# Softmax of a tiled attention: exponentials on ScalarE from PSUM by row groups, with the maximum as bias and the sums accumulated

## The reference

```python
# q, k, v: (8, 8, 576, 64), q and k times 8
k_p = k.reshape(B, H, 72, 8, D).mean(axis=3)
v_p = v.reshape(B, H, 72, 8, D).mean(axis=3)
scores = scale * np.matmul(q, k_p.transpose(0, 1, 3, 2))      # 576 x 72 a head
scores = scores - np.max(scores, axis=-1, keepdims=True)
attn = np.exp(scores)
attn = attn / (np.sum(attn, axis=-1, keepdims=True) + 1e-09)
x = np.matmul(attn, v_p)         # -> (4608, 512), heads side by side
h = x @ w_in;   x = np.maximum(0.01 * h, h) @ w_out           # 512 -> 2048 -> 512
h = x @ w2_in;  out = (h * np.clip(h + 3, 0, 6) / 6) @ w2_out
```

## Time and profile before

| | us |
|---|---|
| median of 3 runs (1792.47 to 1794.03) | 1793.36 |
| the profiled execution, its own time | 1795.66 |
| its span, first to last instruction | 1793.9 |
| TensorE busy | 1713.4 (96%) |
| DVE busy | 1032.4 (58%) |
| ACT busy | 623.1 (35%) |
| GpSimd busy | 696.9 (39%) |

### The profile page before, as it was taken

One profiled execution on the slowest core, in us unless ns is written; L12 is line 12 of the kernel. 1 busy time (PEld: TensorE's weight loads), 2 busy tenths in 40 slices (PEclk: granted clock), 3 DMA queues, 4 the chain that ended last, 5 costly groups with the idle time before them and its releaser, 6 DMA issues. The chain is left out here.

```text
span 1793.9 us, 34434 instructions
## 1 busy us (share of the span) xinstructions
PE 1713.4 (96%) x10794; PEld 1513.2 (84%) x10794; DVE 1032.4 (58%) x1786; ACT 623.1 (35%) x1249; POOL 696.9 (39%) x773
## 2 busy tenths in 40 slices
PE   7888889999999999999999999999999999999999
PEld 7676778888888888888889888988898989888898
DVE  8664755767767677675544555444444444444444
ACT  4443333323333233333222334333433343333333
POOL 5667867666855667522220424120303030312200
PEclk8898999999999999999999999999999999999999
DMA  5744567776867768665757775766666676757562
GB/s 142 236 128 148 186 224 241 249 247 208 272 208 253 231 213 261 214 220 172 223 177 245 213 233 175 214 198 201 202 191 219 176 216 179 219 177 215 176 200 80
DMA packets 218111, 366.81 MB, mean 204 GB/s; under 512 B 22464, under 2 KB 47040, under 8 KB 218048
## 3 DMA queue, kind: packets, MB, share of 16 engines
q1 hardware_dynamic: 218048, 366.04, 65.9%
HBM read 308.28 MB, written 57.67 MB: 204 GB/s over the span
## 5 line engine op out<-in xcount | busy, mean ns | idle before, releaser
L1341 PE MATMUL ps_h<-xs_hi,ring 128*128 128x256 f32 x3808 | 819.3, 283 | 22.6 <-issue 8.5
L1341 PEld LDWEIGHTS ps_h<-xs_hi,ring 128*128 128x128 f32 x3808 | 642.2, 189 | 72.8 <-issue 37.6
L1341 PE MATMUL ps_h<-xs_lo,ring 128*128 128x256 f32 x1904 | 533.7, 280 | 0.0
L1341 PEld LDWEIGHTS ps_h<-xs_lo,ring 128*128 128x128 f32 x1904 | 359.7, 189 | 27.8
L921 ACT ACTIVATE g_hi<-gate 128x512 fp32r<-128x512 f32 x288 | 182.0, 632 | 452.9 <-DVE gate L1101 260.8
L718 POOL TENSOR_TENSOR xs_lo<-x_stage,xs_hi 128x512 fp32r<-128x512 f32 x51 | 74.8, 1466 | 464.3 <-ACT xs_hi L893 464.3
L1134 DVE TENSOR_TENSOR u<-ps_h,p 128x256 f32<-128x256 f32 x272 | 114.5, 421 | 208.4 <-PE ps_h L1341 186.9
L1293 PE MATMUL ps_y<-g_hi,wout_hi 128*128 128x512 f32 x576 | 229.3, 398 | 0.2
L1295 PE MATMUL ps_y<-g_hi,wout_lo 128*128 128x512 f32 x576 | 228.5, 397 | 0.0
L1293 PE MATMUL ps_y<-wout_hi,g_hi 128*128 128x512 f32 x576 | 226.2, 393 | 1.4 <-DVE y_stage L1130 1.4
L1295 PE MATMUL ps_y<-wout_hi,g_lo 128*128 128x512 f32 x576 | 227.0, 394 | 0.0
(11 more groups left out here) (127 smaller groups left out, 2417.9 us busy)
## 6 DMA issues: line engine op xcount, KB each, us to landing
ring<-w_in_split SPq DMA_DIRECT2D x920, 256.0 KB, 2.8
w_in_split<-ring SPq DMA_DIRECT2D x56, 256.0 KB, 4.0
w_in_split<-stage SPq DMA_DIRECT2D x56, 256.0 KB, 3.4
k_raw<-in_kT SPq DMA_DIRECT2D x32, 288.0 KB, 3.7
q_raw<-in_qT SPq DMA_DIRECT2D x32, 288.0 KB, 4.4
v_raw<-in_v SPq DMA_DIRECT2D x32, 288.0 KB
x0T<-x_stage SPq DMA_DIRECT2D x32, 288.0 KB, 4.1
x1T<-y_stage SPq DMA_DIRECT2D x36, 256.0 KB, 3.6
```

Source lines behind the costliest of these rows:

```text
L1341: mm = pe.matmul(banks[BANK_OF[r]], a, b[:, r, c, :], start=r in OPENS and c == 0 and n == 0, stop=c == 1 and n == 2, skip_group_check=True)
```

## The change

Four things. The stage exp is split in two, exp0 and exp1, one for each half, with places of their own. In them ACT reads the scores from PSUM by the six groups of 72 columns, one instruction each, with the negated and scaled maximum as bias (a pointer to one value per row), writes the exponentials to `prob`, and accumulates their sum into `row_sum`. DVE makes the bias (a small multiplication a half) in place of the subtraction, and the two row sums go. And normalize waits for both halves at once; the places of normalize, divide and turn_p0 are moved as the list says, and the wait for the earlier transposes goes from DVE to ACT.

```diff
-STAGES = ("split_qk", "scores", "exp", "normalize", "divide", "turn_p0", "pv0", "turn_p1", "pv1")
-UNIT_PLACES = [(0, 3, 4, 5, 6, 9, 11, 12, 14),
-               (11, 15, 16, 17, 18, 20, 23, 24, 26),
-               (23, 27, 28, 29, 30, 33, 35, 36, 38),
-               (35, 39, 40, 41, 42, 44, 47, 48, 50)]
+STAGES = ("split_qk", "scores", "exp0", "exp1", "normalize", "divide", "turn_p0", "pv0", "turn_p1", "pv1")
+UNIT_PLACES = [(0, 3, 4, 5, 6, 7, 9, 11, 12, 14),
+               (11, 15, 16, 17, 19, 19, 21, 23, 24, 26),
+               (23, 27, 28, 29, 30, 31, 33, 35, 36, 38),
+               (35, 39, 40, 41, 43, 43, 45, 47, 48, 50)]
...
 # FIRST_STAGES: ("exp", c) becomes ("exp0", c), ("exp1", c) in the same place of the list
...
+            u.row_bias = buf("row_bias", [ROWS, 2, HALF_SUB * 2])
...
-                if name == "exp":
-                    for half in range(2):
-                        act.wait_ge(shifted, 2 * n + half + 1)
-                        nc.scalar.activation(u.prob[:, half], u.prob[:, half], ACT.Exp,
-                                             scale=SCORE_SCALE).then_inc(exp_ready, 1)
+                if name in ("exp0", "exp1"):
+                    half = int(name[-1])
+                    act.wait_ge(bias_ready, 2 * n + half + 1)
+                    above_zero(act, p_turned, 2 * freed(b, c))
+                    for r in range(HALF_SUB * 2):
+                        rows_exp = nc.scalar.activation(
+                            u.prob[:, half, r], u.ps[0:ROWS, half, r * KEYS:(r + 1) * KEYS],
+                            ACT.Exp, bias=u.row_bias[:, half, r:r + 1], scale=SCORE_SCALE,
+                            accum_out=u.row_sum[:, half, r:r + 1])
+                    rows_exp.then_inc(exp_ready, 1)
...
-                    above_zero(dve, p_turned, 2 * freed(b, c))
                     for half in range(2):
                         dve.wait_ge(max_ready, 2 * n + half + 1)
-                        nc.vector.tensor_tensor(u.prob[:, half], scores(u, half),
-                                                spread(u.row_max[:, half]), ALU.subtract
-                                                ).then_inc(shifted, 1)
+                        nc.vector.tensor_scalar(u.row_bias[:, half], u.row_max[:, half],
+                                                -SCORE_SCALE, None, ALU.mult
+                                                ).then_inc(bias_ready, 1)
                 if name == "normalize":
-                    for half in range(2):
-                        dve.wait_ge(exp_ready, 2 * n + half + 1)
-                        nc.vector.tensor_reduce(u.row_sum[:, half], u.prob[:, half], AXIS_X,
-                                                ALU.add).then_inc(sum_ready, 1)
-                    dve.wait_ge(sum_ready, 2 * n + 2)
+                    dve.wait_ge(exp_ready, 2 * n + 2)
```

More of the change, by code:

```diff
@@ L80 @@
 STORE2_PLACES = (19, 31)
[L82 to L91, removed]
+FIRST_STAGES = [("sum_k", 0), ("sum_k", 1), ("split_qk", 0), ("split_qk", 1),
+                ("scores", 0), ("exp0", 0), ("exp1", 0), ("scores", 1), ("exp0", 1),
+                ("exp1", 1), ("normalize", 0), ("divide", 0), ("split_qk", 2),
+                ("turn_p0", 0), ("pv0", 0), ("normalize", 1), ("divide", 1), ("round", 0),
[4 rows of a table added]
+                ("normalize", 3), ("divide", 3), ("pv0", 2), ("round", 4), ("round", 5),
+                ("turn_p1", 2), ("turn_p0", 3), ("split_x", 0), ("split_x", 1), ("pv1", 2),
+                ("pv0", 3), ("round", 6), ("round", 7), ("turn_p1", 3), ("split_x", 2),
+                ("pv1", 3), ("split_x", 3)]
 WARM_UP = 8
@@ L231, in ffn_attention_kernel @@
         max_ready = sem("max_ready")
-        shifted = sem("shifted")
+        bias_ready = sem("bias_ready")
         exp_ready = sem("exp_ready")
-        sum_ready = sem("sum_ready")
         den_ready = sem("den_ready")
```

## The result

The changed kernel takes 1822.65 us (median of 3 runs, 1822.01 to 1825.31) against 1793.36 (1792.47 to 1794.03). The ratio is 1.0173, with a 95% interval of 1.0149 to 1.0197: 29.3 us slower, where 53 were forecast. The profiled execution of after took 1822.0 us, that of before 1795.7.

The account below looks back on a forecast made before the run. TensorE, busy 96% of the span, was taken to bound the kernel. Tiles 1 to 6 add 42 us, tile 0 4, before tile 0 7: 53 us on 1795.7, less 2.3, gives 1846 us; range 1789 to 1886.

Parts of the forecast that it names:

- units 1 and 3: Steps 2 and 5 of attention tiles: TensorE delayed 2.4 us each, two per tile, in tiles 1 to 6.
- h late at part 4: Steps 2 and 5: ACT's copy h stands behind exp0, so TensorE's part 4 starts 1.6 us late.
- pv0 behind the upper g_hi: Steps 2 and 5: pT_hi follows g_hi on ACT, so TensorE goes on at pv0 at 678.55 instead of 677.5.
- X: Time from one 96x72 exponential to the next on ACT: 0.44 us taken, bounds 0.24 and 0.54.
- rival A: DVE's relief decides: row sums free on ACT, X 0.24, about 8 us faster, 1785 us; chance 0.13.
- units 0 and 2: Attention tiles 1 to 6: the exponentials make copy p and TensorE's part 2 late, 1.1 us each.
- DVE's relief: Subtractions and row sums go, small multiplications come: DVE gets back 2.0 us per unit, 64 us in all.
- before tile 0: One chain of DVE, ACT and TensorE sets the pace there; ACT's longer exponentials add 7 us.
- tile 0: Delay from turn_p0 to pv0 of units 1 and 3 and later weight splitting: 4 us, between 0 and 10.
- nothing differs: Sign: from tile 7 on, the changed kernel runs as before.
- B: The second instruction, reading the sum, does not overlap: X 0.54 or a little over, 1884 us; chance 0.21.
- C: No change: X near 0.25, GpSimd's stretching merely falls on other instructions, 1793 us; chance 0.08.

Follow-up runs that it names:

- e5: The changed kernel with turn_p0 of units 1 and 3 back at its old place, one position earlier: 1809.47 us, ratio 1.0095.
- e9: The changed kernel with ACT's upper g_hi of steps 2 and 5 put behind pT_hi, as it stood before: 1812.34 us, ratio 1.0133.
- e3: The kernel before, with its own arithmetic, but normalize, divide and turn_p0 at the changed kernel's places: 1821.99 us, ratio 1.0152.
- e4: The changed kernel with exp0 of units 1 and 3 one place later, behind ACT's copy h: 1829.72 us, ratio 1.019.
- e7: The change in units 0 and 2 alone; units 1 and 3 as in the kernel before, arithmetic and places: 1797.07 us, ratio 1.003.
- e1: The kernel before with only the new buffer row_bias added, unused, shifting later allocations by 48 bytes a partition: 1794.64 us, ratio 1.0012.
- e12: The changed kernel itself, run again beside e11 for comparison: 1822.56 us, ratio 1.0184.
- e8: The kernel before without maximum and subtraction, one exponential of 96x432 a half straight from PSUM, sums on DVE: 1774.13 us, ratio 0.991.
- e10: The kernel before with one maximum for all six groups of a half as bias of one exponential from PSUM: 1780.37 us, ratio 0.9945.
- e11: The changed kernel with the first unit's row_bias at the end of the allocation, so other tensors lie as before: 1820.98 us, ratio 1.0174.
- e6: The changed kernel without the accumulator output, row_sum set once to a constant: 1806.07 us, ratio 1.0097.

## Why the prediction was right in kind and nearly twice too large

**Right in place, and in size partly by luck: units 1 and 3.** I put 2.4 us each, from h late at part 4 and pv0 behind the upper g_hi. Measured: steps 2 and 5 longer by 2.11 and 1.77 us in the mean. Both waits are there under the names foretold, h 4.6 to 13.1 us (I said over 20) and pT_lo 24.5 to 36.6 (over 35). e5 and e9 take away one link each of the second (turn_p0's place, g_hi ahead of pT_hi), and pv0's wait goes or shrinks by two thirds. e3 shows that the places make this wait without the new arithmetic, e4 that the two waits belong to one chain: remove the first, and the second takes its length.

The size came out of two errors that offset each other. With X at the measured 0.295, my own working gives part 4 at 670.4, the last exponential at 672.1, pT_lo at 676.8 and about 0.65 us a unit, not 2.4, or some 8 us in tiles 1 to 6. The term that was too small is DVE's: 0.4 us for the two small operations and 1.2 for the division. In after, of the ten places at which these precede pv0 (steps 2 and 5 of tiles 2 to 6), three have no GpSimd instruction beside them; there they take 1.6 us in all, as I put it, and pv0 waits 0.4. At the other seven they take 2.3 to 3.2 us, and pv0 waits 1.1 to 2.1. Before, they were stretched in the same way, but the chain had room, and pv0 waited at none of the ten. I used GpSimd's stretching only for rival A, and not in this chain.

**Wrong: X, and with it units 0 and 2.** The failing term is X, 0.44 foretold, 0.295 measured. I had the right instruction (a second one, of 209 ns; the nearest row had 203), but took it to stand in line with its exponential but for one neighbour's overlap. It overlaps at both ends, and adds only 0.09 us. By my own working, twelve pieces then take 3.5 us instead of 5.3, and p comes before TensorE's part 2 has use for it: units 0 and 2 cost nothing instead of 1.1 each. The wait for p stayed at 2.7 us (I said over 10), steps 1 and 4 did not grow, and e7 has these two units alone at 0.3% with the layout in it. DVE's relief was 52 us in all against my 64, since the 96x6 multiplications took 0.35 us each in the mean and not 0.2. That takes 2.2 x 6 = 13 us off the 53.

**Wrong: before tile 0 and tile 0.** 7 and 4 us foretold, 0.4 measured for both. TensorE's first matmul of tile 0 came 2.2 us late (54.3 against 52.0), and tile 0 gave back 1.8 of it; both are near the scatter (50.6 in e1, 52.1 in e12). The 7 follow X: with 0.295 my working gives about 1 (0.5 each for units 2 and 3). In tile 0 one gain repeats: the longest wait for the divided probabilities is 5.6 us in before, e1 and e3, where row_den took 2.33 to 2.35 us, and 2.8 us in after and e12, where it took 0.17. That is the wait that rival A named. e8 and e10 point the same way: in this stretch less DVE work pays. That this gain nearly cancels ACT's growth is argued; no run divides tile 0 itself.

**Not foreseen: the layout**, about 2 us from tile 7 on. I wrote "nothing differs" there. e1 and e11 show it in the matmuls' rows.

**The sum** by measured terms: 0.4 + 1.6 + 22.1 + 2.2 = 26.3 us in the profiled executions (29.3 in the medians). That the forecast came within a factor of two thus rests on an X that was too large and a DVE chain that was too short. Of the 22.1, (2.11 + 1.77) x 5 = 19.4 are of steps 2 and 5, and the rest falls on the other six. Of that rest step 3 has most (+1.00 in the mean), but in two of its five tiles it is 1.5 us and more over the others, as single steps in before are too, so I read no mechanism from it.

**The rivals.** A (relief of DVE decides) needs X below about 0.25, and the exponentials alone, without sums, are at 0.21 (e6). Still e6 is 1.0097: with the places as they are, even a free sum would have left the kernel slower, so my point from which A decides was wrong, being laid on X alone. Its other half is borne out: the wait of 5.6 us that it named went down to 2.8, and e8 and e10, where ACT hardly grows and the places stay, are faster. B (no overlap) is out by the timeline. C (no change) is out by the interval.

**What stays open:** why 48 bytes of shift cost 4 ns a matmul and 64 bytes more in the step; and how the loss divides exactly between places and arithmetic. e3, e4 and e6 bound it, but they do not add up, since all of them lengthen or shorten one chain, and the lower clock comes with the longest waits. No run takes GpSimd's work away from beside DVE, so that it is the cause of the stretching is read from the traces alone. The new arithmetic with every place as it was before, in all four units, was not run.

## What to carry to other kernels

Pieces of 96x72 of one split exponential stood 0.21 us apart here, and 0.295 with an accumulated sum, so that twelve took 3.5 us where two of 96x432 took 1.1: count it at the place in the queue where it stands, and ask what stands behind it. When a stage is moved by one place, look on every engine for which instruction it now comes after, and for how much work is left before its result is needed; here moving one stage back by one place (e5) gave as much as taking out the accumulated sums (e6), 0.78% and 0.76%. A chain whose room has been used up also pays for every stretching of its members that cost nothing before. When removing one wait moves it along a chain to the next, shorten the chain: the one-bias version (e10) takes work off DVE and puts hardly any on ACT (busy 624.7 us against 623.1).

## What the runs showed of the hardware that I had not expected

- ACTIVATION_READ_ACCUMULATOR takes 209 ns by its row and adds 0.09 us to the distance of two exponentials (0.295 against 0.21).
- Shifting operands in SBUF by 48 bytes a partition takes the matmuls of 256 columns that read `xs_lo` from 279 to 283 ns; by 64 bytes the plain step goes to 10.56 us (10.47 unshifted).
- Small operations on DVE are short when GpSimd has no instruction beside them. In after the 96x12 addition took 169 to 170 ns at all 14 such places, and 479 in the mean at the other 18 (up to 1251); the 96x6 multiplication 162 against 416; a half of the division 600 against 927. The reciprocal between them took 223 to 225 ns at all 32. So my 0.2 held for an undisturbed one, and the means of 349 and 344 mix the two.
- Waits of TensorE of some 2 us in one piece came with a lower granted clock over the whole run: 0.974 to 0.976 in the four runs of e3 and 0.968 to 0.978 in those of e4, against 0.978 to 0.983 in those of after and e12 and 0.982 to 0.986 in those of e5, which waits less.
